# A three-stage kernel whose expert stage gets 25 whole slots and six half slots of rows

## What is computed

```
noisy_logits = x @ w_gate + log1p(exp(x @ w_noise)) * noise
top2   = two largest of noisy_logits per row;  top2_w = softmax over the two
for e in range(8):
    for k in range(2):
        mask = top2[:, k] == e
        h = maximum(x[mask] @ w1[e], 0)
        out[mask] += top2_w[mask, k, None] * (h @ w2[e])
```

## Time and profile before

| | |
|---|---|
| median of three runs | 1195.03 us |
| the profiled execution's own time | 1196.79 us |
| its span | 1195.0 us |
| mean granted TensorE clock | 0.949 |
| TensorE busy | 1036.7 us (87%) |
| VectorE busy | 887.2 us (74%) |
| ScalarE busy | 618.1 us (52%) |
| GpSimd busy | 468.4 us (39%) |
| DMA, mean | 140 GB/s, 226 to 243 GB/s in the expert stage |

### The profile page before, as it was taken

The page is one execution under the profiler, slowest core; times in us unless marked ns, Lnnn a source line. Parts: engine busy times, 40 slices in busy tenths (PEclk is TensorE's granted clock), DMA queues, the critical chain, the costliest instruction groups (busy, mean ns, idle before and its releaser), DMA issues.

```text
span 1195.0 us, 21893 instructions
## 1 busy us (share of the span) xinstructions
PE 1036.7 (87%) x7866; PEld 979.6 (82%) x7866; DVE 887.2 (74%) x1729; ACT 618.1 (52%) x967; POOL 468.4 (39%) x417
## 2 busy tenths in 40 slices
PE   0036898998898899989947999999999999999996
PEld 0035797897797798878847999999999999999996
DVE  6888989988989989845554776776767777677672
ACT  6354555754754745534533555555555555555551
POOL 4122232443543533344532434434543543453442
PEclk9987899898899899989977999999999999999998
DMA  9420130230130121211406676776667667676640
GB/s 255 154 78 21 44 104 27 58 96 28 55 100 27 47 55 38 58 34 54 126 15 212 215 252 227 247 241 231 248 225 263 248 217 248 216 253 221 218 152 1
DMA packets 85980, 167.51 MB, mean 140 GB/s; under 512 B 18566, under 2 KB 57696, under 8 KB 85872
## 3 DMA queue, kind: packets, MB, share of 16 engines
q1 hardware_dynamic: 72432, 137.71, 35.9%
q0 software_dynamic: 13440, 28.40, 6.5%
HBM read 148.83 MB, written 21.92 MB: 143 GB/s over the span
## 4 chain that ended last, share of the span: by engine, by line
PE 61%; DVE 3%; issue 2%; ACT 1%; DMA 1%; POOL 0%; POOLq 0%; another core or an unknown queue 0%; DVEq 0%; ACTq 0%; SPq 0%
PE bank L1387 22%; PE bank L1567 22%; PE bank L1431 4%; PE bank L1479 4%; PE bank L1378 3%; PE bank L1453 2%; PE bank L1491 1%; PE bank L1497 1%; PE bank L1511 1%; PE bank L1468 0%; DVE zl L1212 0%; DVE w1l L1098 0%; DVE turn L999 0%; DMA xg<-xs,mine 0%; PE bank L1407 0%
## 5 line engine op out<-in xcount | busy, mean ns | idle before, releaser
L911 ACT ACTIVATE hh<-bank 128x256 fp32r<-128x256 f32 x248 | 95.3, 384 | 255.8 <-PE bank L1387 254.8
L1387 PE MATMUL bank<-sxh,w1h 128*128 128x256 f32 x744 | 212.0, 285 | 2.1 <-DVE sxl L1337 2.1
L1387 PE MATMUL bank<-sxh,w1l 128*128 128x256 f32 x744 | 210.3, 283 | 0.0
L1387 PE MATMUL bank<-sxl,w1h 128*128 128x256 f32 x744 | 210.0, 282 | 0.0
L1356 DVE SCALAR_TENSOR_TENSOR hl<-bank,hh 128x256 fp32r<-128x256 f32 x248 | 104.8, 423 | 120.1 <-ACT hh L911 110.0
L681 POOL DMA_INDIRECT out<-yo,mine x62 | 78.0, 1259 | 276.8 <-DVE yo L1349 267.4
L1567 PE MATMUL bank<-w2h,hh 128*128 128x384 f32 x496 | 167.2, 337 | 0.0
L1567 PE MATMUL bank<-w2l,hh 128*128 128x384 f32 x496 | 166.6, 336 | 0.0
L1567 PE MATMUL bank<-w2h,hl 128*128 128x384 f32 x496 | 166.4, 335 | 0.0
L1387 PEld LDWEIGHTS bank<-sxh,w1h 128*128 128x128 f32 x744 | 140.6, 189 | 2.5 <-DVE sxl L1337 2.5
L1387 PEld LDWEIGHTS bank<-sxh,w1l 128*128 128x128 f32 x744 | 141.5, 190 | 0.0
(11 more groups left out here) (196 smaller groups left out, 2445.7 us busy)
## 6 DMA issues: line engine op xcount, KB each, us to landing
raw<-in_w SPq DMA_DIRECT2D x62, 1536.0 KB
ar<-in_a_re SPq DMA_DIRECT2D x6, 768.0 KB, 4.6
turn<-in_a_im SPq DMA_DIRECT2D x6, 768.0 KB, 6.3
qk<-in_q SPq DMA_DIRECT2D x48, 96.0 KB, 2.3
qk<-in_k SPq DMA_DIRECT2D x48, 96.0 KB, 2.4
out<-wide SPq DMA_DIRECT2D x9, 512.0 KB, 11.8
vt<-in_v SPq DMA_DIRECT2D x24, 192.0 KB, 2.6
xs<-x SPq DMA_DIRECT2D x24, 192.0 KB, 2.7
```

Source lines behind the costliest of these rows:

```text
L911: nc.scalar.activation(hh[:, f % NH, :], bank[:, f % 2, 0:CAP], ACT.Relu).then_inc(hh_done, 1)
L1387: ins = MM(dst, stationary[a_](cc), moving[b_](cc), start=(n_ == 0), stop=(n_ == len(terms) - 1))
```

## The change

The table is counted in units of 128 rows. Slots 5, 10, 15, 20, 25 and 30 become half slots of 128 rows; the other 25 remain whole. Their number stays 31. An expert's full 256s (and remainders over 128) go to whole slots, a remainder of up to 128 to a half one. The table takes 24 dependent steps instead of 14, and GpSimd writes its constants with eight iotas instead of two.

In a half slot the roles of the first product are exchanged: 128 tokens are stationary and 512 columns of w1 move, in two parts, one per PSUM bank. The hidden rows then lie with tokens on partitions, so ScalarE writes them rectified to `row_h`, TensorE turns them in two groups of four, ScalarE copies the turned result to `hh` and VectorE makes the remainder `hl`. Weights come in two raw buffers instead of one, by parity. In front of a half slot, w1 of the slot behind it is converted at the end of the whole slot before; w2 of the slot behind it is converted within the half slot.

```
-SLOTS = (2 * NTOK - (E - 1)) // CAP + E
+WHOLE, HALVES = 25, 6
+SLOTS = WHOLE + HALVES
+HALF_SLOTS = (5, 10, 15, 20, 25, 30)
...
             def load_w1(s):
-                e = sp.value_load(slot_expert[0:1, bass.ds(s, 1)], min_val=0, max_val=E - 1)
-                apart(sp, (w1_lo, KC * s))
-                sp.dma_start(raw1[:], w1[bass.ds(e, 1)]...).then_inc(raw1_loaded, 16)
+                e = sp.value_load(slot_expert[0:1, bass.ds(table_row(s), 1)], min_val=0, max_val=E - 1)
+                apart(sp, (w1_lo, KC * (s - 1)))
+                sp.dma_start(raw1[s % 2][:], w1[bass.ds(e, 1)]...).then_inc(raw1_loaded[s % 2], 16)
...
             def partial(s, par, k):
-                wait(pool, y_sent, 32 * s)
-                wait(pool, y2_evac, 2 * (s - 1))
+                wait(pool, y_sent, 16 * units_upto(s - 1))
+                wait(pool, y2_evac, units_upto(s - 2))
...
-                for u in range(SUB):
+                for u in range(units(s)):
...
```

ScalarE's half slot:

```
+                row(0)
+                if more:
+                    tokens(s + 1, 1 - par)
+                row(1)
+                high(0)
+                high(1)
+                if more:
+                    for j_ in range(W2P):
+                        w2_piece(s + 1, 1 - par, j_)
```

VectorE, at the end of a whole slot and in a half slot:

```
+                if is_half(s + 1) and s + 2 < SLOTS:
+                    for cc in range(KC):
+                        w1_piece(s + 2, par, cc)
...
+            def half_slot(s, par, more):
...
+                if more:
+                    tokens(s + 1, 1 - par)
+                low(0)
+                low(1)
+                give(s - 1, 1 - par, (s - 1) % NM)
+                if more:
+                    for j_ in range(W2P):
+                        w2_piece(s + 1, 1 - par, j_)
```

TensorE:

```
+            def half_hidden(s, par, part):
...
+                cols = slice(512 * part, 512 * (part + 1))
+                split_product(bank[:, part, :],
+                              (lambda cc: sxh[par][:, cc, 0:P], lambda cc: sxl[par][:, cc, 0:P]),
+                              (lambda cc: w1h[par][:, cc, cols], lambda cc: w1l[par][:, cc, cols]), KC, h2_mm)
...
+            def half_slot(s, par, more):
+                if more:
+                    tokens(s + 1, 1 - par)
+                half_hidden(s, par, 1)
+                half_turn(s, par, 0)
+                half_turn(s, par, 1)
+                if more:
+                    first_hidden(s + 1, 1 - par)
+                half_result(s, par, 0)
+                half_result(s, par, 1)
```

More of the change, by code:

```diff
@@ L51, with is_half, table_row, units @@
 LN_LIMIT = math.log(0.999)
+def is_half(s):
+    return s in HALF_SLOTS
+def table_row(s):
+    return WHOLE + HALF_SLOTS.index(s) if is_half(s) else s - sum(t < s for t in HALF_SLOTS)
+def units(s):
+    return 1 if is_half(s) else SUB
+def units_upto(s, step=1):
+    return sum(units(t) for t in range(s, -1, -step))
+def steps(s):
+    return sum(2 if is_half(t) else FC for t in range(s))
 def wait(eng, sem, value):
@@ L320, in solu_moe_program, with turn_bank @@
         turned = bank[:, 4:6, :].rearrange("p b x -> p (b x)")[:, 0:KC * CAP]
+        turned_half = turned[:, 0:KC * P].rearrange("p (c t) -> p c t", t=P)
+        hh_half = hh[:].rearrange("p r (k t) -> p (r k) t", t=P)
+        hl_half = hl[:].rearrange("p r (k t) -> p (r k) t", t=P)
+        def turn_bank(par, part):
+            return Y_BANK[par] + 1 if part == 0 else 1
         def part(t, q):
@@ L1312, in _, with over @@
             one = slice(0, 1)
-            count, slots, upto = cnt[:, 0, :], cnt[:, 1, :], cnt[:, 2, :]
+            count, whole, any_, odd, pairs_upto, odd_upto, odd_ahead = (cnt[:, i_, :] for i_ in range(7))
             by_slot = [1, SLOTS, E]
+            def over(x):
+                return x[one].unsqueeze(1).to_broadcast(by_slot)
             then(V.scalar_tensor_tensor(out=count, in0=expert_no[:], scalar=-float(REGION), in1=rank_base[:],
                                         op0=ALU.mult, op1=ALU.add))
-            then(V.tensor_tensor(fills[:], count.unsqueeze(2).to_broadcast([P, E, MAXS]), thresh[:], ALU.is_gt))
@@ L1332, in _ @@
-            then(V.tensor_copy(tail_row[:], rank_base[one]))
+            for i_ in range(2):
+                then(V.tensor_tensor(fills[:, i_], count.unsqueeze(2).to_broadcast([P, E, MAXS]), thresh[:, i_], ALU.is_gt))
+            then(V.tensor_reduce(cnt[:, 1:3, :], fills[:], AX.X, ALU.add))
+            then(V.tensor_tensor(odd, any_, whole, ALU.subtract))
+            then(V.tensor_tensor_scan(pairs_upto, ones[:, 0:E], whole, 0.0, ALU.mult, ALU.add))
+            then(V.tensor_tensor_scan(odd_upto, ones[:, 0:E], odd, 0.0, ALU.mult, ALU.add))
@@ new lines, in _ @@
+            then(V.tensor_tensor(odd_ahead, odd_upto, odd, ALU.subtract))
+            in_pairs, in_odd = (slot_cmp[:, i_] for i_ in range(2))
+            own = in_pairs
+            at_pair, at_odd = (x[:].unsqueeze(2).to_broadcast(by_slot) for x in (pair_no, odd_no))
+            then(V.tensor_tensor(in_pairs, over(pairs_upto), at_pair, ALU.is_le))
+            then(V.tensor_reduce(slot_f[:, 0, :], in_pairs, AX.X, ALU.add))
+            then(V.tensor_tensor(in_pairs, in_pairs, over(whole), ALU.mult))
@@ L1551, in expert_hidden @@
                     pe.wait_ge(w1_lo, KC * (s + 1))
-                wait(pe, hl_done, FC * s + f - 1)
+                if f == 0 and s > 0 and is_half(s - 1):
+                    pe.wait_ge(row_done, 2 * HALF_SLOTS.index(s - 1) + 1)
+                else:
+                    wait(pe, hl_done, steps(s) + f - 1)
                 cols = slice(f * P, (f + 1) * P)
```

244 lines of the change are left out of this document (161 added, 83 removed).

## The result

The changed kernel takes **1201.31 us** (median of 4 runs, 1200.75 to 1203.66), the kernel before 1194.78 us on the same chip (4 runs). The ratio is 1.0059, with a 95% interval of 1.0042 to 1.0077: slower by 0.6%, where 0.7% and 1203.4 us were forecast. The profiled execution took 1200.75 us; its span of 1198.6 us is 3.6 us longer than the one before. The stage computes 7168 rows where it computed 7936, and the time did not fall.

The account below looks back on a forecast made before the run. TensorE was taken to bound the expert slots, 17.55 us each. From the median of 1195.03 us, -44.1 + 35 + 12.5 + 5 = +8.4 us gave 1203.4 us, range 1180 to 1213.

Parts of the forecast that it names:

- The half slot's own work: TensorE in six half slots: 10.2 us each instead of 17.55, a gain of 44.1 us for six.
- Idle time: TensorE waits for the third hl behind five half slots, held by prev's late landing: 7.0 us each, 35 us.
- The clock: TensorE's granted clock falls after each of five idle gaps, costing 2.5 us each, 12.5 us in all.
- The end: Last slot is a half one whose yo waits for scatter and prev after TensorE ends: +5 us.
- The table's 24 steps and the added iotas: Longer table on VectorE (about 3.7 us) and more GpSimd iota fall into idle or waiting time: costed at nothing.
- Prev lands early: Rival: behind half slots the gather lands before or beside the weights, 3.1 us; 1191 or 1179 us. Chance 0.27.
- The chain gets longer: Rival: in half slots GpSimd waits on VectorE's w2 subtractions, about 1.5 us each, 1211 us. Chance 0.15.
- No stall at all: Rival: VectorE's or GpSimd's order takes prev off the path in half slots, 1156 us. Chance 0.08.

Follow-up runs that it names:

- run 12: Changed kernel with half slots 4, 9, ... 29, yo spread over three slots, and every slot's weight loads held until prev has landed: 1151.45 us, ratio 0.9626.
- run 2: Changed kernel with yo of the slot before made ahead of both hidden-row subtractions in the half slot: 1185.78 us, ratio 0.9924.
- run 10: Changed kernel with only the weight loads of the slot three behind a half slot held until the half slot's prev landed: 1188.82 us, ratio 0.9934.
- run 5: Changed kernel with yo of the slot before made earlier in half slots, and weight loads behind a half slot's gather held until prev landed: 1157.23 us, ratio 0.9688.
- Run 11: Changed kernel with half slots 4, 9, ... 29 (last slot whole), yo spread over three slots, loads held in three slots around each half one: 1158.08 us, ratio 0.9685.
- run 3: Changed kernel with 24 unread filler matmuls of 512 columns in TensorE's idle time in slots behind a half one: 1196.96 us, ratio 1.001.
- run 6: Changed kernel with yo of the half slot at step 5 of the next slot instead of step 1: 1196.88 us, ratio 1.0021.
- run 1: Changed kernel with half slots' rows stored without adding what out already holds, so their yo waits for no gather: 1168.38 us, ratio 0.9782.
- run 9: Changed kernel with one raw buffer each for w1 and w2, as before the change: 1202.29 us, ratio 1.005.

## Why the prediction was right

**The half slot's own work: -44.1 us.** Nine matmuls of 512 columns took 2.09 us, or 0.23 each, as forecast from another part of the program. The rest is read from TensorE in run 12, half slot 4: from the first turn of hidden rows to the product behind the turns, and the first and last of the 24 output matmuls with what follows.

```profile
715.83 0.60 PE L1512 MATMUL bank<-ident,row_h 128*128 128x128 f32 x4
716.67 0.66 PE L1512 MATMUL bank<-ident,row_h 128*128 128x128 f32 x4 [0.25 <-ACT row_h L985]
717.09 0.36 PE L1521 MATMUL bank<-sxh,w1h 128*128 128x256 f32 x1
...
718.24 0.34 PE L1733 MATMUL bank<-w2h,hh 128*128 128x384 f32 x1
...
722.23 0.33 PE L1733 MATMUL bank<-w2h,hl 128*128 128x384 f32 x1
722.41 0.28 PE L1521 MATMUL bank<-sxh,w1h 128*128 128x256 f32 x1
```

Turns and their wait are 1.26 us, the output 4.17, the hidden products 2 x 2.09 and the tokens' transposes some 0.65: 10.3 us, against 10.2 in the forecast. As a whole, run 12 has the half slots almost without waits and is 3.7% faster than before, 44.7 us of 1194.9. Its expert stage is 506.5 us long where the kernel before has 549.9, 43.5 us less. So the gain was there, at about its forecast size, and the five waits took it back. Whole slots kept their length: scatters at 659.81 and 677.36 are 17.55 us apart.

**Idle time: 35 us forecast, 35.2 measured.** The place, the instruction that ends it and the number of times are as forecast, and on the mean of the five places the terms are too. From `yo` of the slot before to the issue of `prev` it was 9.45, 8.46, 9.47, 9.06 and 8.45 us, 8.98 on the mean, for 8.6 forecast. The landing of `prev` was 5.25 us on the mean for 5.5. From there to TensorE's first matmul it was 2.36 for 2.15, and TensorE had work for 12.35 us (slot 5) for 12.05.

In the single places the forecast is less good. In slots 5 and 15 the scatter took 4.6 us to land, not the 3.4 of the earlier trace rows, so `prev` was issued 0.9 us later than worked out; and then it took 4.3 to 4.5 us and not 5.5. In slots 10 and 25 the scatter had landed after 3.0 us and the gather took 6.2. So errors of a microsecond cancel in part within the places and between them, and no run shows that they must: that the sum came out to 0.2 us is luck. The forecast put the loads just ahead of the gather; they went out 0.15 to 0.59 us behind it. Runs 2 and 10 show that this order decides 2 us or more in either direction.

**The clock: 12.5 us forecast.** The low clock held for 23.4 us in the five places. Half of it is lost, 11.7 us. That this is a cost of its own, beside the idle time, is read from the length of the expert stage, which is 554.1 us in the changed kernel. In run 10 it is 539.2: 14.9 us less, for 14.6 us less idle time, with all five falls left. In run 5, where the clock no longer fell, it is 514.9: 39.2 us less, for 28.0 us less idle time and the clock's 11.7. The rest of run 5's 44 us is 2.6 us at the end (10.5 us instead of 13.1 from the last matmul on), and what lies ahead of the stage and between executions.

**The end: +5 us forecast, +1.8 measured.** This term was mis-sized. From the last matmul to the end of the span it was 11.3 us before (1183.68 to 1195.0) and is 13.1 now (1185.46 to 1198.6). The landings in the chain at the end:

```profile
1185.01 2.12 DMA out<-yo,mine
...
1187.95 2.60 DMA prev<-out,mine
...
1190.67 0.63 DVE yo L1451
```

The scatter landed in 2.12 us, not 3.4, and `prev` in 2.60, not 3.1. From TensorE's end to the last `yo` being done it was 5.8 us, where 7.3 were forecast. From there to the end of the span it is 7.3 us, and was 10.2 before: the scatter less gave back 2.9 us, where 1.3 were taken. The two errors add up to 3 us. Run 11 was built on the mis-sized term and accordingly gained nothing.

**Sum.** Forecast -44.1 + 35 + 12.5 + 5 = +8.4. Measured: the stage from its first transposes of tokens to the last matmul is 554.1 us instead of 549.95, +4.15. With 35.2 of idle time and 11.7 of the clock in it, -42.7 are left for the six half slots, 1.4 us short of the forecast. The end is +1.8; the stage began 2.4 us earlier, which lies within what executions differ by there (629.1 to 636.7 us over these runs). That is the 3.6 us of the two spans, and the medians differ by 6.5. Against these measured terms the forecast had the end 3.2 us and the clock 0.8 us too dear, and the half slots' gain 1.4 us too large. The table's 24 steps and the added iotas cost nothing that can be seen.

**The rivals.** *Prev lands early* is what the gather does with the loads held back: 2.1 to 2.6 us in run 10. In the changed kernel it took 4.26 to 6.19, above the 3.9 us from which the case would have been faster. The Trainium skill, "DMA: Bandwidth & Descriptors", section "Queues, rings and completion order", lets each engine take turns between its queues. The forecast made an estimate of about 4 us from it, and the 4.26 and 4.52 of two places are near that. The 5.12 to 6.19 of the other three and the 5.50 to 8.08 of run 2 do not agree with it. *The chain gets longer*: the scatter issued under the w2 subtractions took 1.80 us (734.25) and the next one 1.41. From `yo` to the second scatter it was 4.07 us, where the earlier trace rows have 3.47: 0.6 us longer in slots 5, 10, 15 and 25. In slot 20 the second scatter was issued a further 1 us later (1007.25), yet its `prev` not later than in slot 5. *No stall at all* came only by edits, at 1151 to 1158 us for the 1156 worked out.

What stays open is how the chip shares its DMA engines so that a load costs a gather 2 to 6 us: the runs show the durations, and nothing of the mechanism. The filler's place (run 3) leaves open what length of idle time lets the clock fall.

## What to carry to other kernels

When a stage's unit of work is made smaller, look for the serial chains that don't shrink with it. Here a scatter to DRAM, its landing, a gather and its landing take about 14 us (13.8 to 14.8 from one `yo` to the next), which a slot of 17.55 us hid and one of 10.2 us did not. Moving one consumer only moves such a wait into the next unit (run 6). What helps is to start the chain earlier, to let its lag out over several units, and to keep large prefetches behind the small gather that someone waits for; here one call moved and one wait added (run 5) turned a loss of 0.6% into a gain of 3.1%, and the whole of it (run 12) into 3.7%.

## What the runs showed of the hardware

The same gather of 128 rows landed in 2.1 to 2.6 us with the weight loads held back (run 10), in 4.3 to 6.2 us with a load issued 0.6 to 0.15 us behind it (the changed kernel), and in 6.4 to 8.1 us with one 0.4 us ahead of it (four places of run 2; in the fifth the load went out 0.2 us behind, and it was 5.50). With a load issued between two gathers the second took 7.68 us (run 1). A scatter landed in 2.12 us at the quiet end, in 3.0 to 4.6 us in the stage, and in 6.1 to 7.5 us with a load issued within a microsecond of it (runs 1, 5 and 9).

The granted clock fell behind an idle time of as little as 1.9 us (run 3, slot 6), yet 3.19 us in the same run (slot 11) and up to 2.2 us in run 5 left it at 1.00. Behind the five waits of the changed kernel it was at the low level already when TensorE restarted; in run 3 TensorE restarted at full clock, and the clock fell 0.4 to 1.5 us later. After a restart it stayed low for 3.0 (run 1) to 6.2 us (run 10). So the idle time alone doesn't tell what follows.
